# A fused kernel of linear attention and two MLPs: the decay chain laid out as fourteen steps of one slot, with ScalarE's cast of the hidden activations put ahead of it

## The chip, the cores and the metric

The kernel runs on one core of a Trainium2 chip, as one program with one instruction stream for each engine: PE (TensorE) multiplies matrices, DVE (VectorE), ACT (ScalarE) and POOL (GpSimd) work on rows of 128 partitions, and SP (SyncE) here only starts DMAs. The streams meet at semaphores. The metric is the device time of one execution in microseconds. Three runs of the kernel before gave 1022.08 us in the median (1019.12 to 1023.35).

## The reference

Three stages, all in fp32. The first is a recurrence over 768 tokens for 4 batches of 8 heads with a 48 x 48 state:

```python
mag = np.sqrt(a_re * a_re + a_im * a_im)
scale = np.minimum(mag, 0.999) / (mag + 1e-06)
a_re_n, a_im_n = (a_re * scale, a_im * scale)
for t in range(S):
    new_re = ar * S_re - ai * S_im
    new_im = ar * S_im + ai * S_re
    S_re, S_im = (new_re + kv, new_im)          # kv: outer product of k[t] and v[t]
    y[:, :, t] = np.einsum('bhd,bhde->bhe', q[:, :, t], S_re)
...
h = x @ w_in;  g = h * np.clip(h + 3.0, 0.0, 6.0) / 6.0;  x = g @ w_out      # 384 -> 2048 -> 384
a = x @ w1;  b = x @ w2;  out = ((a * b) @ w3) @ w_out2                       # 384 -> 1024 -> 1024 -> 384
```

## The kernel before, in words

**Units.** The 3072 tokens are 24 chunks of 128; three chunks are a unit of 384 tokens, so there are eight units (NU = 8) and six chunks to a batch. The recurrence is done by chunk: the decays of a token are turned into a magnitude and an angle, both are summed along the tokens, and q and k are multiplied by the exponential of the one sum and by the cosine and sine of the other. After that the scores of a chunk, its output y and the state's update are plain matrix products.

**Slots.** The first MLP sets the beat. A unit u >= 0 has sixteen slots, one for each 128 columns of the hidden layer (n = 16u + slot). In a slot PE does `gemm1(n)` (nine products into the bank `hb`), then `gemm2(n-2)` (nine products into `acc`). For each n ACT makes `t_sb` from `hb` (relu), DVE makes `g_sb`, ACT casts it to its high part `gH` (`high_g`), and POOL subtracts to get the low part `gL` (`low_g`). gemm2(n) needs both parts, gemm1(n+2) needs `g_sb` of n to have been made. `t_sb` and `g_sb` are single buffers; gH and gL have three.

**What rides on the slots.** Units -2 and -1 have no MLP work and fill the pipeline. The chunks of unit u+1 are treated in unit u, in three stages each: TK (PE transposes the rotated keys of a chunk; ACT and DVE copy them to `Kc` and `Ks`), S (`Sc`: scores from the tile `F`; DVE masks them) and YU (PE makes y and the state's update; ACT and DVE split y into high and low; SP stores it to `xHL`, six DMAs by L707 to L712). From unit 1 on they stand in slots 1, 5, 9 (TK), 2, 6, 10 (S) and 4, 8, 12 (YU). The last chunk of a batch has no TK and no update; it falls into the even units. The decay chain `pre(p, t)` of unit p, with t the step, is done in unit p-2: `steps(u, sl)` says which steps stand in which slot. It ends with `QKc` and `QKs`, q and k times the cosine and the sine. SP then scatters them by head into `F` with ten DMAs for the first two chunks (`scatter_pair`) and ten for the third (`scatter_last`, which writes where the first chunk stood).

**Order within a slot.** All engines walk the same two loops, and each does its slot's work in the order in which the code has it: an engine that waits holds up all that stands behind it, SP's DMAs too. On ACT, before: relu, the chain's step, `high_g`, the chunk's copies, the splits of weights. On DVE: `g_sb`, the chain's step, the chunk's work.

**Also in the pipeline's filling.** PE multiplies w3 by w_out2 in unit -2 (L890); ACT copies the eight blocks of rows out (`W3_COPY`) and SP stores them. The weights of the first MLP are split into high and low parts in eight pieces (`SPLIT_H` on ACT, `SPLIT_L` on POOL). In unit 7 the weights of the second MLP are split, each 3072 columns wide, on ACT (L1081) and DVE (L1279). After it comes the second MLP, which the change doesn't touch.

## Time and profile before

| | |
|---|---|
| median of three runs | 1022.08 us |
| the profiled execution, and its span | 1022.37 us, 1020.6 us |
| busy share of PE, DVE, ACT, POOL | 89%, 46%, 42%, 25% |
| mean granted TensorE clock | 0.946 of full speed |
| PE waited for F<-QKs, in total and times | 26.8 us, 8 |
| PE waited for POOL's gL in gemm2, in total and times | 23.6 us, 10 |

A busy share counts an instruction from its start to its end, and products overlap, so a high share of PE doesn't say that it runs at its best rate. What counts is the distance from one slot's first product to the next one's, against the same kind of slot where nothing was waited for. Everything else is read as lateness against that beat.

### The profile page before, as it was taken

How to read it: one execution, taken by the hardware profiler on the slowest of the kernel's cores; microseconds unless marked ns; L12 is line 12 of the kernel's file. 1: busy time of each engine (PE TensorE's matmuls, PEld its weight loads, DVE VectorE, ACT ScalarE, POOL GpSimd, SP SyncE). 2: the span in 40 equal slices, each digit the busy share in tenths (PEclk: the TensorE clock that was granted, in tenths of full speed). 3: DMA queues.
4: the chain of work that ended last, by engine and by line, in shares of the span. 5: the costliest groups of instructions: out<-in, count | busy, mean ns of one | idle time of the engine just before them, and what ended most of it. 6: DMA issues, size and time to landing. Idle time of an engine off the chain costs nothing.

```text
span 1020.6 us, 14665 instructions
## 1 busy us (share of the span) xinstructions
PE 910.4 (89%) x5721; PEld 834.9 (82%) x5721; DVE 470.5 (46%) x610; ACT 430.5 (42%) x650; POOL 256.6 (25%) x200
## 2 busy tenths in 40 slices
PE   6944469889989989989989989989999999999996
PEld 3534468879889889889889889989888888888886
DVE  6445549849658648648748733233212121212110
ACT  4543535555655655555555532353212122212121
POOL 1011336222222222222222222343222222222221
PEclk9977769989989999999999999999999999999999
DMA  9584132353343343343344141510101010101000
GB/s 347 201 230 128 46 63 78 85 119 88 108 87 95 100 91 98 93 90 99 107 89 110 48 84 50 188 68 11 44 1 62 1 62 1 62 1 62 1 32 33
DMA packets 73688, 85.85 MB, mean 84 GB/s; under 512 B 6928, under 2 KB 59792, under 8 KB 73616
## 3 DMA queue, kind: packets, MB, share of 16 engines
q1 hardware_dynamic: 73216, 84.07, 29.7%
q10 hardware_dynamic: 400, 0.80, 0.5%
q8 instruction: 48, 0.79, 0.3%
q14 instruction: 24, 0.20, 0.1%
HBM read 45.22 MB, written 11.01 MB: 55 GB/s over the span
## 4 chain that ended last, share of the span: by engine, by line
issue 39%; PE 38%; POOL 14%; DVE 3%; ACT 2%; DMA 2%; SPq 1%; ACTq 0%; POOLq 0%; DVEq 0%
POOL gL L1328 13%; PE hb L937 10%; PE acc L959 7%; PE bQ L937 5%; PE bR L937 5%; PE bP L959 2%; PE hb L796 2%; PE acc L816 2%; PE acc L890 2%; DMA F<-QKs 1%; PE hb L890 1%; DVE QKc L1198 1%; DMA wo_sb<-in_moe_w_out_dram 1%; PE bQ L846 0%; PE bR L846 0%
## 5 line engine op out<-in xcount | busy, mean ns | idle before, releaser
L1328 POOL TENSOR_TENSOR gL<-g_sb,gH 128x384 fp32r<-128x384 f32 x128 | 157.1, 1227 | 428.2 <-ACT gH L1036 425.9
L796 PE MATMUL hb<-xHL,winH 128*128 128x384 f32 x768 | 168.6, 356 | 10.7 <-DMA xHL<-yHL 9.1
L816 PE MATMUL acc<-gH,woutH 128*128 128x384 f32 x384 | 134.0, 349 | 32.5 <-POOL gL L1328 23.6
L1237 DVE SCALAR_TENSOR_TENSOR g_sb<-t_sb,hb 128x384 f32<-128x384 f32 x128 | 70.4, 550 | 189.6 <-ACT t_sb L1046 105.8
L796 PEld LDWEIGHTS hb<-xHL,winH 128*128 128x128 f32 x768 | 140.2, 199 | 13.3 <-DMA xHL<-yHL 9.5
L1046 ACT ACTIVATE t_sb<-hb,cst 128x384 f32<-128x384 f32 x128 | 74.4, 581 | 154.1 <-PE hb L796 153.4
L816 PE MATMUL acc<-gH,woutL 128*128 128x384 f32 x384 | 133.3, 347 | 0.0
L816 PE MATMUL acc<-gL,woutH 128*128 128x384 f32 x384 | 132.8, 346 | 0.0
L1341 POOL TENSOR_TENSOR pL<-p_sb,pH 128x512 fp32r<-128x512 f32 x48 | 67.0, 1396 | 231.9 <-ACT pH L1098 231.9
L816 PEld LDWEIGHTS acc<-gH,woutH 128*128 128x128 f32 x384 | 75.0, 195 | 37.6 <-issue 29.3
L1036 ACT CAST gH<-g_sb 128x384 fp32r<-128x384 f32 x128 | 65.3, 510 | 79.4 <-DVE g_sb L1237 79.2
L796 PE MATMUL hb<-xHL,winL 128*128 128x384 f32 x384 | 88.9, 339 | 0.0
L816 PEld LDWEIGHTS acc<-gH,woutL 128*128 128x128 f32 x384 | 75.4, 196 | 0.0
L816 PEld LDWEIGHTS acc<-gL,woutH 128*128 128x128 f32 x384 | 75.2, 196 | 0.0
L1090 ACT COPY a_sb<-hb 128x512 f32<-128x512 f32 x48 | 28.1, 586 | 102.7 <-PE hb L937 102.7
L796 PEld LDWEIGHTS hb<-xHL,winL 128*128 128x128 f32 x384 | 70.4, 192 | 0.0
L1296 DVE TENSOR_TENSOR p_sb<-a_sb,bQ 128x512 f32<-128x512 f32 x24 | 16.5, 688 | 110.2 <-PE bQ L937 94.4
L1098 ACT CAST pH<-p_sb 128x512 fp32r<-128x512 f32 x48 | 29.8, 621 | 85.5 <-DVE p_sb L1296 85.5
L1296 DVE TENSOR_TENSOR p_sb<-a_sb,bR 128x512 f32<-128x512 f32 x24 | 16.5, 686 | 104.7 <-PE bR L937 99.7
L846 PE MATMUL bQ<-F 128*128 128x128 f32 x192 | 32.5, 323 | 28.2 <-DMA F<-QKs 26.8
L846 PEld LDWEIGHTS bQ<-F 128*128 128x128 f32 x192 | 29.3, 228 | 31.9 <-DMA F<-QKs 29.7
L959 PE MATMUL acc<-woH,pL 128*128 128x384 f32 x144 | 48.7, 338 | 0.0
(148 smaller groups left out, 1715.9 us busy)
## 6 DMA issues: line engine op xcount, KB each, us to landing
QKs<-in_qk_x_dram SPq DMA_DIRECT2D x16, 576.0 KB, 4.2
xHL<-yHL SPq DMA_DIRECT2D x48, 144.0 KB, 2.7
F<-QKc SPq DMA_DIRECT2D x16, 292.5 KB, 4.7
AR<-in_a_re_x_dram SPq DMA_DIRECT2D x8, 576.0 KB, 3.9
...
```

Source lines behind the costliest of these rows:

```text
L796: mm = pe.matmul(o, w[:, kk * DF1 + ft * P:kk * DF1 + (ft + 1) * P], xv(u)[:, 2 * kk + part, :], start=(i == 0), stop=(i == 8))
L816: mm = pe.matmul(acc[m][:, 0:UNIT], w[:, ft * DM + m * P:ft * DM + (m + 1) * P], gg[:, (n % 3) * UNIT:(n % 3 + 1) * UNIT], start=(ft == 0 ...
L846: mm = pe.matmul(bk[:, hh * P:(hh + 1) * P], qk(f_of(g))[:, b, P:2 * P], qk(f_of(g))[:, b, 0:P], start=True, stop=True)
L890: mm = pe.matmul(w3_banks[i % nb][:, 0:DM], w3t_sb[:, j * DF2 + i * P:j * DF2 + (i + 1) * P], wo2_sb[:, j * DM:(j + 1) * DM], start=(j == ...
L937: mm = pe.matmul(bk[n % 2][:, :], w[:, kk * DF2 + ft * P:kk * DF2 + (ft + 1) * P], x[:, o:o + UNIT2], start=(i == 0), stop=(i == 8))
L959: mm = pe.matmul(acc2[tb][:, 0:DM], pp[:, o:o + P], w[:, ft * DM:(ft + 1) * DM], start=(ft == 0 and i == 0), stop=(ft == FT2 - 1 and i == 2))
L1036: act.copy(gH[:, (n % 3) * UNIT:(n % 3 + 1) * UNIT], g_sb[:, :]).then_inc(s["hswish_high"], 1)
L1046: act.activation(t_sb[:, :], hb[n % 2][:, 0:UNIT], ACT.Relu, bias=THREE_C).then_inc(s["relu_done"], 1)
L1237: dve.scalar_tensor_tensor(out=g_sb[:, :], in0=t_sb[:, :], scalar=6.0, in1=hb[n % 2][:, 0:UNIT], op0=ALU.min, op1=ALU.mult).then_inc(s["hs ...
L1296: dve.tensor_tensor(p_sb[:, (n % 2) * UNIT2:(n % 2 + 1) * UNIT2], a_sb[:, (n % 2) * UNIT2:(n % 2 + 1) * UNIT2], bb[n % 2][:, :], ALU.mult) ...
L1328: pool.tensor_tensor(gL[:, (n % 3) * UNIT:(n % 3 + 1) * UNIT], g_sb[:, :], gH[:, (n % 3) * UNIT:(n % 3 + 1) * UNIT].bitcast(F32), ALU.subt ...
L1341: pool.tensor_tensor(pL[:, (n % 3) * UNIT2:(n % 3 + 1) * UNIT2], p_sb[:, (n % 2) * UNIT2:(n % 2 + 1) * UNIT2], pH[:, (n % 3) * UNIT2:(n % ...
```

## The change

- **Steps.** The chain has fourteen steps (t = 0 to 13) in place of sixteen. From unit 1 on step t stands in slot t; slots 14 and 15 are empty. Work that an engine needs from the other one is made one slot earlier. The angle's arctangent is now at t = 6, ahead of the exponentials at t = 9, so that ACT changes its function table four times a chain, not three. The multiplication by 1/pi moves from ACT into three DVE instructions. A fourth work buffer `W4` is the room of `gH` for p < 2 and `x_sb` (x2_sb) after that, with waits that protect both.
- **Pair and last.** q and k of a unit are loaded, decayed and rotated in two portions: the first two chunks (`pair`), then the third (`last`). `scatter_pair` is issued for cosine and sine at t = 13, all of it from SP; before, at t = 14 and t = 15, and for p = 0 one half from ACT.
- **Loads.** The decay rows of the next unit (`load_a`) are asked for at t = 11, not t = 12 (slot 11 in place of slot 12 from unit 1 on).
- **ACT's order.** `high_g(n)` stands right behind the relu, ahead of the chain's step.
- **Splits.** The weight pieces are split in another order and other slots (`SPLIT_W`); w3's rows are copied out earlier; the splits in unit 7 are done in halves, one a slot.

```diff
-        SPLIT_H = {(-1, 0): (0,), (-1, 8): (4,), (-1, 9): (1,), (0, 1): (5,), (0, 3): (2,), (0, 5): (6,), (0, 7): (3,), (0, 9): (7,)}
+        SPLIT_W = {(-2, 15): (0,), (-1, 3): (1,), (-1, 8): (4,), (0, 0): (2,), (0, 2): (5,), (0, 4): (3,), (0, 6): (6,), (0, 8): (7,)}
...
             if u == -1:
-                return ([(1, 0)] if sl == 0 else []) + ([(1, sl + 1)] if sl < 9 else [])
+                return [(1, sl)] if sl <= 10 else []
             if u == 0:
-                return {0: [(1, 10), (1, 11)], 1: [(1, 12), (1, 13)], 2: [(1, 14), (1, 15)],
-                        3: [(2, 0), (2, 1)], 15: [(2, 13), (2, 14), (2, 15)]}.get(sl, [(2, sl - 2)])
-            return [(u + 2, sl)] if u + 2 < NU else []
+                return {15: [(2, 12), (2, 13)]}.get(sl, [(2, sl - 3)] if sl >= 3 else [(1, sl + 11)])
+            return [(u + 2, sl)] if u + 2 < NU and sl < 14 else []
...
-        W3_COPY = {(-2, 9): (0, 1), (-2, 10): (2,), (-2, 11): (3, 4), (-1, 0): (5,), (-1, 1): (6,), (-1, 2): (7,)}
+        W3_COPY = {(-2, 8): (0, 1), (-2, 9): (2,), (-2, 10): (3, 4), (-2, 14): (5, 6), (-2, 15): (7,)}
...
         def evac_x2_act(act, u):
...
+            act.wait_ge(s["turns_wrapped"], min(u + 3, NU))
...
         @block.sync
...
-                        if t == 12 and p + 1 < NU:
+                        if t == 11 and p + 1 < NU:
                             load_a(p + 1)
-                        if t == 14:
+                        if t == 13:
                             scatter_pair(sp, p, 0)
-                        if t == 15 and p > 0:
                             scatter_pair(sp, p, 1)
...
         @block.scalar
...
+                if t == 3:
+                    if p > 2:
+                        act.wait_ge(s["x2_stored"], 16 * KT * (p - 2))
+                    act.activation(W4(p)[:, :], W1[:, :], ACT.Exp, scale=-0.5).then_inc(s["exp_ln_mag"], 1)
...
+                if t == 6:
+                    act.wait_ge(s["atan_arg"], p + 1)
+                    act.activation(W2[:, :], W2[:, :], ACT.Arctan, scale=-1 / QUARTER_TURN).then_inc(s["atan_done"], 1)
+                if t == 9:
                     act.wait_ge(s["log_r_centred"], p + 1)
                     act.activation(mid_decay[:, :], blocks(W1)[:, :, P // 2 - 1], ACT.Exp).then_inc(s["mid_decays"], 1)
-                if t == 9:
-                    act.wait_ge(s["atan_num"], p + 1)
                     act.activation(AI[:, :], AR[:, :], ACT.Exp).then_inc(s["q_decays"], 1)
                     act.activation(AR[:, :], AR[:, :], ACT.Exp, scale=-1.0).then_inc(s["k_decays"], 1)
                 if t == 10:
-                if t == 12:
-                    act.wait_ge(s["turns_summed"], KT * (p + 1))
-                    act.mul(W2[:, :], W1[:, :], float(1 / np.pi)).then_inc(s["turns"], 1)
-                if t == 13:
                     act.wait_ge(s["turns_wrapped"], p + 1)
...
                         act.activation(t_sb[:, :], hb[n % 2][:, 0:UNIT], ACT.Relu,
                                        bias=THREE_C).then_inc(s["relu_done"], 1)
+                        high_g(n)
                         if sl == 1 and u > 0:
                             evac_x2_act(act, u - 1)
-                    if n is not None:
                         for p, t in steps(u, sl):
                             pre(p, t)
-                        high_g(n)
...
         @block.vector
...
                 if t == 12:
+                    dve.wait_ge(s["pair_decayed"], 2 * (p + 1))
                     dve.wait_ge(s["cos_turns"], p + 1)
                     for i in range(2):
-                        dve.tensor_tensor(part(QKc, i), part(QKs, i), tokens(W3), ALU.mult).then_inc(s["cos_rotated"], 1)
-                if t == 15:
+                        dve.tensor_tensor(pair(part(QKc, i)), pair(part(QKs, i)), pair(tokens(W2)), ALU.mult).then_inc(s["pair_cos"], 1)
...
-                    if u == NU - 1 and sl in (5, 7, 9):
+                    if u == NU - 1 and 4 <= sl < 10:
```

What this makes of the engines' order is shown at three places. First ACT in unit -2, the chain of unit 0 (W_64 and W_65 are work buffers, x_sb the place of w3's rows). Before:

```order
L1007 ACTIVATE W_64<-W_64 128x1152
L1010 ACTIVATE mid_decay<-W_63 128x9
L1013 ACTIVATE AI<-AR 128x1152
L1014 ACTIVATE AR<-AR 128x1152
L1075 COPY x_sb<-acc 128x384 x2
L1017 ACT_TABLE_LOAD
L1017 ACTIVATE W_64<-W_64 128x1152
L1075 COPY x_sb<-acc 128x384
```

and after it:

```order
L1022 ACTIVATE W_65<-W_65 128x1152
L1025 ACT_TABLE_LOAD
L1025 ACTIVATE W_65<-W_65 128x1152
L1086 COPY x_sb<-acc 128x384 x2
L1028 ACT_TABLE_LOAD
L1028 ACTIVATE mid_decay<-W_64 128x9
L1029 ACTIVATE AI<-AR 128x1152
L1030 ACTIVATE AR<-AR 128x1152
L1086 COPY x_sb<-acc 128x384
```

The arctangent (L1017, now L1025) has moved ahead of the first copies of w3's rows, and the two exponentials behind them, with a table load of their own. Second ACT in a steady unit. Before, slots 12 and 13 with the chain's end:

```order
L1020 ACTIVATE W_64<-W_63 128x1152
L1036 CAST gH<-g_sb 128x384
L1067 CAST yHL<-bP 128x4x128
L1046 ACTIVATE t_sb<-hb,cst 128x384
L1023 ACTIVATE W_64<-W_63 128x1152
L1025 ACT_TABLE_LOAD
L1025 ACTIVATE W_64<-W_63 128x1152
L1026 ACTIVATE W_64<-W_63 128x1152
```

After, slot 9 and the beginning of slot 10, the widest piece of the new chain:

```order
L1058 ACTIVATE t_sb<-hb,cst 128x384
L1048 CAST gH<-g_sb 128x384
L1028 ACT_TABLE_LOAD
L1028 ACTIVATE mid_decay<-W_64 128x9
L1029 ACTIVATE AI<-AR 128x1152
L1030 ACTIVATE AR<-AR 128x1152
L1070 COPY Kc<-bQ 128x288
L1071 COPY Kc<-bQ 128x2x32
L1072 COPY Kc<-bQ 128x2x16
L1058 ACTIVATE t_sb<-hb,cst 128x384
L1048 CAST gH<-g_sb 128x384
```

The cast to gH stood behind all of the chain's step and now stands ahead of it; the key copies Kc stand behind it in both. Third SP at the end of unit 1, the last chunk's stores (xHL), the decay rows (AR, AI) and the scatter. Before:

```order
L662 DMA v_sb_72<-in_v_dram 128x384
L707 DMA xHL<-yHL 48x6x128
L708 DMA xHL<-yHL 48x6x128
L709 DMA xHL<-yHL 32x2x128
L710 DMA xHL<-yHL 32x2x128
L711 DMA xHL<-yHL 16x2x128
L712 DMA xHL<-yHL 16x2x128
L640 DMA AR<-in_a_re_x_dram 128x1152
L640 DMA AI<-in_a_im_x_dram 128x1152
L338 DMA F_68<-QKc 48x2x780
```

and after it:

```order
L650 DMA AR<-in_a_re_x_dram 128x1152
L650 DMA AI<-in_a_im_x_dram 128x1152
L673 DMA v_sb_73<-in_v_dram 128x384
L720 DMA xHL<-yHL 48x6x128
L721 DMA xHL<-yHL 48x6x128
L722 DMA xHL<-yHL 32x2x128
L723 DMA xHL<-yHL 32x2x128
L724 DMA xHL<-yHL 16x2x128
L725 DMA xHL<-yHL 16x2x128
L347 DMA F_69<-QKc 48x2x780
```

The decay rows now go ahead of the last chunk's stores; the scatter stands directly behind these stores.

## Rows read from the trace of the kernel before

**Rows 1.** Windows, by unit: length, busy PE, PEld, DVE, ACT, POOL, clock, DMA share, GB/s

```profile
101.53:202.67 101.14, 74.21 (x490) 70.13 (x490) 67.80 (x76) 52.14 (x70) 40.84 (x22) 0.83 0.27 66
202.67:280.76 78.09, 70.64 (x531) 67.73 (x532) 51.07 (x68) 46.33 (x70) 18.66 (x16) 0.93 0.41 107
280.76:355.96 75.20, 69.39 (x509) 66.91 (x509) 51.79 (x68) 41.71 (x63) 20.19 (x17) 0.94 0.39 96
355.96:431.53 75.57, 70.08 (x531) 67.66 (x531) 51.37 (x69) 42.19 (x66) 19.29 (x16) 0.95 0.38 95
...
581.62:651.90 70.28, 67.07 (x509) 65.65 (x509) 24.19 (x41) 21.27 (x44) 16.57 (x16) 0.97 0.29 64
651.90:708.00 56.10, 51.95 (x287) 50.87 (x287) 18.98 (x20) 25.52 (x37) 23.63 (x16) 0.97 0.29 109
```

**Rows 2.** Timeline of PE, unit 2: first products of slots 4 to 7

```profile
302.47 1.20 PE L796 MATMUL hb<-xHL,winH 128*128 128x384 f32 x6
...
308.50 1.31 PE L796 MATMUL hb<-xHL,winH 128*128 128x384 f32 x6
...
312.30 1.29 PE L796 MATMUL hb<-xHL,winH 128*128 128x384 f32 x6
...
317.21 1.29 PE L796 MATMUL hb<-xHL,winH 128*128 128x384 f32 x6
```

**Rows 3.** Timeline of PE across the boundary of units 1 and 2

```profile
279.12 0.41 PE L816 MATMUL acc<-gH,woutH 128*128 128x384 f32 x1 [2.10 <-POOL gL L1328]
...
280.76 1.20 PE L796 MATMUL hb<-xHL,winH 128*128 128x384 f32 x6
...
283.88 1.20 PE L796 MATMUL hb<-xHL,winH 128*128 128x384 f32 x6
...
291.86 0.41 PE L816 MATMUL acc<-gH,woutH 128*128 128x384 f32 x1 [2.06 <-ACT gH L1036]
...
295.99 2.07 PE L846 MATMUL bQ<-F 128*128 128x128 f32 x8 [1.25 <-DMA F<-QKs]
```

**Rows 4.** Timeline of ACT, slot 13 of unit 1

```profile
272.47 1.28 ACT L1025 ACT_TABLE_LOAD   x1
273.77 1.26 ACT L1025 ACTIVATE W<-W,cst 128x1152 f32<-128x1152 f32 x1
...
277.39 0.51 ACT L1036 CAST gH<-g_sb 128x384 fp32r<-128x384 f32 x1
```

**Rows 5.** Timeline of DVE, slots 12 and 15 of unit 1

```profile
268.59 2.14 DVE L1188 TENSOR_TENSOR W<-W,W 128x1152 f32<-128x1152 f32 x1
...
283.38 3.43 DVE L1202 TENSOR_TENSOR QKs<-QKs,W 128x1152 f32<-128x1152 f32 x2
```

**Rows 6.** Timeline of SP, first and last of the ten scatters

```profile
283.02 0.60 SPq L338 DMA_DIRECT2D F<-QKc  x1
...
290.81 0.59 SPq L342 DMA_DIRECT2D F<-QKs  x1
```

**Rows 7.** Timelines of ACT, PE, SP and DVE, units -2 to 0

```profile
34.15 0.48 ACT L1075 COPY x_sb<-acc 128x384 f32<-128x384 f32 x1 [7.62 <-PE acc L890]
...
62.54 2.08 PE L846 MATMUL bQ<-F 128*128 128x128 f32 x8 [9.05 <-DMA F<-QKs]
63.83 7.41 SPq L697 DMA_DIRECT2D w3o_dram<-x_sb  x2
...
101.53 2.29 PE L796 MATMUL hb<-xHL,winH 128*128 128x384 f32 x6 [6.11 <-DMA xHL<-yHL]
...
124.16 5.84 DVE L1198 TENSOR_TENSOR QKc<-QKs,W 128x1152 f32<-128x1152 f32 x2
...
142.98 1.44 PE L846 MATMUL bQ<-F 128*128 128x128 f32 x5 [3.94 <-DMA F<-QKs]
```

**Rows 8.** Timelines of POOL and PE in unit 7

```profile
681.29 3.50 POOL L1328 TENSOR_TENSOR gL<-g_sb,gH 128x384 fp32r<-128x384 f32 x1 [3.28 <-ACT gH L1036]
...
684.93 0.66 PE L816 MATMUL acc<-gH,woutH 128*128 128x384 f32 x1 [2.38 <-POOL gL L1328]
```

More of the change, by code:

```diff
@@ L259, in rows_of, with half @@
             return t[:, :].rearrange("p (c j n) -> p j c n", j=KT, n=QK)
+        def half(t, i):
+            n = N1 // 2
+            return t[:, i * n:(i + 1) * n]
         def hd(t):
@@ L719, in _ @@
                 if j == 3:
[L720 to L721 removed]
+                    load_pair(0)
+                    load_last(0)
             for i in range(2):
@@ L753, in _ @@
                         load_x2(0)
-                    if u == NU - 2 and sl == 15:
+                    if u == NU - 2 and sl == 13:
                         for i in range(2):
@@ L1075, in _ @@
                         act.copy(x2_sb[:, (i % 3) * DM:(i % 3 + 1) * DM], w3_banks[i % len(w3_banks)][:, 0:DM]).then_inc(s["w3_row_copied"], 1)
-                    for i in SPLIT_H.get((u, sl), ()):
+                    for i in SPLIT_W.get((u, sl), ()):
                         split_H(act, i)
-                    if u == NU - 1 and sl in (4, 6, 8):
-                        i = sl // 2 - 2
+                    if u == NU - 1 and 3 <= sl < 9:
+                        i, part2 = divmod(sl - 3, 2)
                         act.wait_ge(s[f"mlp2_w_dma{i}"], 16)
-                        act.copy(w2parts[i][0][:, :], w2parts[i][2][:, :]).then_inc(s["mlp2_w_high"], 1)
+                        act.copy(half(w2parts[i][0], part2), half(w2parts[i][2], part2)).then_inc(s["mlp2_w_high"], 1)
             split_x2_act(act, 0)
@@ L1166, in pre @@
                     dve.tensor_copy(fs, fc).then_inc(s["f_column"], 1)
-                if t == 10:
-                    dve.wait_ge(s["q_decays"], p + 1)
-                    dve.wait_ge(s["q_dma"], 16 * (p + 1))
-                    dve.tensor_tensor(part(QKs, 0), part(QKs, 0), tokens(AI), ALU.mult).then_inc(s["q_decayed"], 1)
+                    dve.wait_ge(s["k_decays"], p + 1)
+                    dve.wait_ge(s["pair_dma"], 16 * (p + 1))
+                    for i, grow in enumerate((AI, AR)):
+                        dve.tensor_tensor(pair(part(QKs, i)), pair(part(QKs, i)), pair(tokens(grow)), ALU.mult).then_inc(s["pair_decayed"], 1)
@@ L1193, in pre @@
-                if t == 14:
-                    dve.wait_ge(s["q_decayed"], p + 1)
-                    dve.wait_ge(s["k_decayed"], p + 1)
+                    dve.wait_ge(s["last_dma"], 16 * (p + 1))
+                    for i, grow in enumerate((AI, AR)):
+                        dve.tensor_tensor(last(part(QKs, i)), last(part(QKs, i)), last(tokens(grow)), ALU.mult).then_inc(s["last_decayed"], 1)
+                if t == 12:
+                    dve.wait_ge(s["pair_decayed"], 2 * (p + 1))
                     dve.wait_ge(s["cos_turns"], p + 1)
@@ new lines, in pre, with pair @@
+                if t == 13:
+                    dve.wait_ge(s["last_decayed"], 2 * (p + 1))
+                    for i in range(2):
+                        dve.tensor_tensor(last(part(QKc, i)), last(part(QKs, i)), last(tokens(W2)), ALU.mult).then_inc(s["last_cos"], 1)
+                    for i in range(2):
+                        dve.tensor_tensor(last(part(QKs, i)), last(part(QKs, i)), last(tokens(W3)), ALU.mult).then_inc(s["last_sin"], 1)
+            def pair(v_):
+                return v_[:, :, 0:2, :]
@@ L1204, in part, with last @@
+            def last(v_):
+                return v_[:, :, 2, :]
             def part(t_, i):
@@ L1336, in _ @@
                         low_g(n)
-                    for i in SPLIT_L.get((u, sl), ()):
+                    for i in SPLIT_W.get((u, sl), ()):
                         split_L(pool, i)
```

172 lines of the change are left out of this document (87 added, 85 removed).

## The prediction, made before the changed kernel ran

> **What bounds the kernel now.** I read the windows by unit first [rows 1]. Each row is one unit of sixteen slots: its length, the busy time of each engine, the granted clock as a share of full speed. The rows are those of units 0 to 3, 6 and 7; units 4 and 5 read like 2 and 3. Unit 0 takes 101 us, units 1 to 5 some 75 to 78, unit 6 70, unit 7 56. PE is busy for nine tenths of a steady unit, yet DVE for 51 us and ACT for 42 of some 75: neither is full, so what is lost is lost to lateness, not to capacity.
>
> How much is lost I read off PE's beat [rows 2]. A slot with YU lasts 308.50 - 302.47 = 6.03 us, one with TK 3.80, one with S 4.91; a plain one 283.88 - 280.76 = 3.12 [rows 3]. Seven plain slots and three of each other kind give 21.8 + 44.2 = 66.1 us. In the even units one chunk has no TK (0.7 us) and no state update, which I estimate at 0.9 of YU's 2.9 us: 64.5. Against [rows 1] the loss is 12.0 us in unit 1, 10.7 in unit 2, 9.5 in unit 3, some 10 and 9.5 in units 4 and 5, 5.8 in unit 6: 57.5 us. Unit 7 has no riders, so 49.9 us would do, against 56.1: 6 us.
>
> Where it is lost stands in [rows 3]: gemm2 waits 2.10 us for gL at the end of unit 1 and 2.06 us for gH in slot 1 of unit 2, and S in slot 2 waits another 1.25 us for F. The clock is 0.93 to 0.95 in these units against 0.97 in units 6 and 7 [rows 1]: after these waits PE works a while at the lower level, and that goes with the loss.
>
> The first wait is ACT's order: a table load at 272.47, cosine, sine, a second load, and only at 277.39 the cast to gH [rows 4]. The last one is SP's: the rotation by the sine begins at 283.38 [rows 5], the ten scatters go from 283.02 to 291.40 (8.4 us), and F is there 4.6 us after that, at 295.99 [rows 6, 3].
>
> In the pipeline's filling [rows 7], ACT sits idle 7.6 us until w3's first row is summed, with unit 0's arctangent behind it; F comes at 62.54; SP then stands 7.4 us at w3's last stores with scatter_last and the x store queued behind; gemm1 starts at 101.53; the first score of unit 0 has its F at 142.98.
>
> **The change, part by part, in units 1 to 6.** *Cast first.* The two waits for gL and gH go, each with its stretch of lower clock. What is late next is the chain itself: ACT now waits in each slot for g before it may start its step, some 0.6 us (relu's end to DVE's end).
>
> *Scatter.* Before, the scatter began 2.3 us into slot 0 of the next unit, 9.4 + 2.3 = 11.7 us after slot 13 began. Now pair's rotations stand in slot 12. From slot 13's start: DVE done with them at +2.7, with y's low half at +3.3, six x stores as on any chunk (0.65 us apart) until +7.2, ten scatters +15.6, landed +20.2. S in slot 2 wants F at 5 x 3.12 + 3.80 = +19.4. So F is 0.8 us late rather than hidden by a wide margin, and it moves with DVE's lateness. I take 1.5 us with clock, from 0 to 4.
>
> *Chain work in ten dense slots.* DVE's chain is about as long as before and now lies in slots 3 to 10 and 12. A two-input product of 1152 columns takes 1.35 us alone and 2.14 beside POOL's gL [rows 5]. Taking 0.75 for a one-input instruction and 2.7 for three scans, as estimates from that 1.35, the chain's work in slots 4 to 8 is 3.5 + 2.7 + 3.4 + 2.7 + 2.9 = 15.2 us, the chunks' some 5 and g 2.4, with up to 4 for POOL: 23 to 27 us, where PE's beat takes 6.03 + 3.80 + 4.91 + 3.12 + 6.03 = 23.9. So DVE may be 0 to 3 us late in slot 9.
>
> *Slot 9 of the odd units.* From slot 9's start: nine products 1.6, relu 0.6, g 0.55, cast 0.5, that is +3.3; then table load 1.28 [rows 4], a short exponential 0.2, two long ones 2.3, key copies 0.7: +7.8. S in slot 10 wants the copies at 3.80 + 3.12 = +6.9. That is at least 0.9 us late; with DVE's lateness up to 4. I take 3.5 us with the lower clock that follows. The even units have no TK there and are spared. This fourth table load is new: it takes 1.28 us, and the next instruction starts 1.30 us after it began [rows 4]. The Trainium skill (ScalarE: Activation LUTs, What ACT_TABLE_LOAD costs) puts a switch at 1.28 us plus 1.38 us of draining, 2.66 us; the row shows nothing of the second part. By the page the copies would come 1.4 us later, 4 us more over three odd units.
>
> So a steady odd unit should last 66.1 + 5 = 71 us, an even one 64.5 + 2.5 = 67, unit 6 67. Unit 1 is worse: its chain's last steps (2, 12) and (2, 13) still share slot 15 of unit 0, DVE needs 5.3 us for them, F lands some 14 us into unit 1 and is wanted at 10: 66.1 + 6 + 3.5 = 75.6. Gains: 2.5 + 8.2 + 4.5 + 7.5 + 4.5 + 3.3 = **30.5 us**.
>
> **Unit 7.** While DVE splits 3072 columns POOL's gL takes 3.50 us, and PE waits 2.38 us for it [rows 8]; two more such places cost less. A half takes half as long and one gL fits behind it in each slot: g 0.5, half split 1.7, gL 1.0 is 3.3 us a slot against 3.12, six times, inside the buffers' slack. I take **5 us** of the 6. By the Trainium skill (SBUF — State Buffer, Who interferes with whom) whichever of the two starts first holds the shared ports for the whole instruction; the row fits, and it is also why more DVE instructions in the dense slots can hold up gL.
>
> **Filling.** Unit 0's chain: the arctangent is out of the way before ACT's 7.6 us of idleness; from 34.15 follow two row copies, load, exponentials (38.9), abs, load, cosine (43.2), copies, sine (45.3). SP can start scattering at 45.0, but all ten go from one queue: 53.2, landed 57.8 against 62.54. 4.7 us earlier. PE's w3 products end at 52 and don't stand in the way. Unit -1: w3's stores no longer stand ahead of scatter_last, so x of chunk 0 is stored 8 us earlier; DVE's steps stand between key copies and masks and give back 1.5: gemm1 starts at about 95, **6.6 us** earlier. Unit 0: before, the cosine product took 5.84 us for two, behind POOL's weight piece [rows 7], and F came 41.5 us after gemm1 began. Now the arctangent, exponentials and cosine of unit 1 precede relu(0); sine, load and one weight piece follow; DVE's pair rotations start at 107, wait for POOL's piece split at 106 (3.4 us), end at 114; scatters until 119.6, landed 124.3 in place of 142.98: 18.7 us earlier in all, **12.1 us** beyond gemm1's 6.6. The rest of unit 0 gains perhaps **2 us**.
>
> **Sum.** 30.5 + 5 + 6.6 + 12.1 + 2 = 56.2 us. The span 1020.6 becomes 964.4; the profiled execution's own time was 1.8 us above its span: 966. That execution took 1022.37 us, the median is 1022.08, so 966 stands as it is.
>
> **Costs at nothing.** ACT's wait in slot 3 for x2_stored: x2 is copied out in slot 1 and stored in slot 2, on HBM some 5 us later, about when slot 3's step begins. SP has ended its scatters at +15.6, and slot 1 begins at +12.5, so the store could be 3 us late; then ACT is, with relu(4) behind it, and still inside the slack of some 3 us between gL and gemm2. The load of the decay rows is needed five slots on.
>
> **Rivals.** *(B) The lateness only moves.* DVE runs over in slots 4 to 9, key copies and F both come 3 to 4 us late with stretches of lower clock, and units 1 to 6 gain under 12 us. For it: DVE's 51 us in a 66 us unit, in bursts; a margin for F of less than nothing. Against: before, slots 3 to 12 kept the beat with nearly the same load. Then 1022 - 12 - 5 - 15 = 990, from 980 to 1002. *(C) All of it goes.* Units 1 to 6 within 1.5 us of the beat, unit 1 within 5: gain 57.5 - 12.5 = 45, and 5 + 25 besides: 947, from 938 to 952. For it: before, the late engine always caught up in the plain slots. *(D) Slower.* With the cast first, the loop relu, g, gH, ACT's step, next relu contains DVE's step as well whenever DVE is late, since ACT may not start its step before g. Were both steps fully in series, a unit would take 1.64 x 16 = 26 us for the loop, some 27 of ACT's and some 45 of DVE's work: 98 us in place of 75, 23 more in each of five units, 1022 - 32 + 115 = 1105. It decides from the point where units 1 to 6 lose over 32 us together, 5 a unit, that is where a third of the two engines' work no longer overlaps. Against: PE's gemm1 gives relu its input two slots ahead of need. *(E) No change worth the name*: filling and steady units cancel.
>
> **Chances.** Forecast (952 to 979) 0.60, B 0.18, C 0.15, D 0.04, E 0.03. The forecast's unknowns are the key copies (0.9 to 4 us, three times), F (0 to 4 us, six times), DVE in unit 0 (6 us either way). For 8 in 10 I take most of C's upper half and B's lower half: 946 to 988. Faster by over 0.5%, which is about what a measurement of this kernel can tell from no change, 0.94; within 0.5% 0.02; slower 0.04.
>
> **What would show it.** Right: slots 15 and 1 of the units without a wait for gL or gH; the scatters beginning about 7 us into slot 13; F no more than 2 us late in slot 2; a wait for Kc in slot 10 in units 1, 3 and 5 and none in 2 and 4; F at about 58 and 124 us; gemm1 at 95; unit 7 under 52 us; no POOL gL over 2 us there. Wrong: waits for gL in slots 9 to 12 (B), ACT waiting for x2_stored in slot 3, units of over 76 us (D), or units 2 and 4 at 65 (C).

## The result, and the profile after

Four runs of the changed kernel gave 983.14 us in the median (982.52 to 984.38), beside 1022.27 us for the kernel before: a ratio of 0.9624, 95% interval 0.9600 to 0.9647. It is 39 us faster; 56 were forecast. The profiled execution took 984.38 us with a span of 982.5.

The windows by unit, cut at gemm1's first products as [rows 1] are; the last row runs to the first product of the second MLP:

```profile
100.08:192.04 91.96, 72.17 (x491) 68.41 (x491) 69.00 (x84) 53.78 (x71) 39.34 (x21) 0.87 0.29 72
192.04:267.16 75.12, 68.67 (x530) 66.05 (x531) 58.07 (x82) 41.62 (x65) 19.95 (x16) 0.98 0.44 112
267.16:338.18 71.02, 67.14 (x509) 63.46 (x509) 53.60 (x73) 41.56 (x63) 20.46 (x17) 1.00 0.40 101
338.18:410.24 72.06, 67.01 (x530) 64.38 (x530) 53.18 (x75) 42.22 (x66) 20.08 (x17) 1.00 0.40 101
...
554.45:620.86 66.41, 65.19 (x508) 63.77 (x509) 20.18 (x38) 21.31 (x44) 16.12 (x17) 1.00 0.32 69
620.86:674.05 53.19, 53.19 (x307) 52.89 (x307) 21.26 (x25) 28.07 (x43) 22.66 (x17) 1.00 0.30 113
```

Against the starts of the units before, the gains are 1.45 us up to gemm1's start (6.6 forecast), 9.2 in unit 0 (14.1 forecast), 3.0, 4.2, 3.5, 3.2, 2.7 and 3.9 in units 1 to 6 (2.5, 8.2, 4.5, 7.5, 4.5, 3.3), and 6.6 in unit 7 (5), where the same stretch took 711.71 - 651.90 = 59.81 us before.

PE's waits, whole program (what PE waited for, from whom: us in total, times, longest):

```profile
PE bQ L859 <- DMA F<-QKs: 23.6, 8, 8.1
...
PE hb L809 <- DMA xHL<-yHL: 11.6, 5, 5.6
...
PE hb L809 <- DVE g_sb L1261: 7.8, 4, 2.6
PE bQ L859 <- ACT Kc L1072: 7.7, 5, 1.8
...
PE acc L829 <- POOL gL L1352: 1.4, 1, 1.4
```

The waits for gL, 23.6 us before, are gone but for one, and others have grown: for g itself (1.6 us before), for Kc (1.0), for the x store (9.1). At the end of unit 2 they look like this (timeline of PE, slots 13 to 15 of unit 2, slot 0 and S in slot 2 of unit 3; the counterpart of [rows 3]):

```profile
324.74 1.33 PE L809 MATMUL hb<-xHL,winH 128*128 128x384 f32 x6
...
328.18 1.31 PE L809 MATMUL hb<-xHL,winH 128*128 128x384 f32 x6
...
333.53 1.33 PE L809 MATMUL hb<-xHL,winH 128*128 128x384 f32 x6 [1.72 <-DVE g_sb L1261]
...
338.18 1.33 PE L809 MATMUL hb<-xHL,winH 128*128 128x384 f32 x6 [0.91 <-DMA xHL<-yHL]
...
349.83 1.16 PE L859 MATMUL bQ<-F 128*128 128x128 f32 x8 [1.30 <-DMA F<-QKs]
```

Slots 14 and 15 last 5.35 and 4.65 us where 3.12 would do. Behind it stand these rows of ACT, slots 9 to 12 of unit 2 (for [rows 4]):

```profile
309.92 0.59 ACT L1058 ACTIVATE t_sb<-hb,cst 128x384 f32<-128x384 f32 x1 [1.03 <-PE hb L809]
313.57 0.51 ACT L1048 CAST gH<-g_sb 128x384 fp32r<-128x384 f32 x1 [3.06 <-DVE g_sb L1261]
314.10 1.28 ACT L1028 ACT_TABLE_LOAD   x1
315.40 0.22 ACT L1028 ACTIVATE mid_decay<-W 128x9 f32<-128x9 f32 x1
...
317.63 0.56 ACT L1058 ACTIVATE t_sb<-hb,cst 128x384 f32<-128x384 f32 x1
...
326.95 0.58 ACT L1058 ACTIVATE t_sb<-hb,cst 128x384 f32<-128x384 f32 x1
```

and these of DVE, the rotations of the pair in slot 12, y's low half and g(13) (for [rows 5]), and of SP, the first and the last scatter (for [rows 6]):

```profile
312.99 0.55 DVE L1261 SCALAR_TENSOR_TENSOR g_sb<-t_sb,hb 128x384 f32<-128x384 f32 x1
...
328.04 2.64 DVE L1209 TENSOR_TENSOR QKc<-QKs,W 128x768 f32<-128x768 f32 x2
330.61 1.81 DVE L1212 TENSOR_TENSOR QKs<-QKs,W 128x768 f32<-128x768 f32 x2
332.34 0.68 DVE L1290 TENSOR_TENSOR yHL<-bP,yHL 128x512 fp32r<-128x512 f32 x1
332.94 0.53 DVE L1261 SCALAR_TENSOR_TENSOR g_sb<-t_sb,hb 128x384 f32<-128x384 f32 x1
```

```profile
337.01 0.60 SPq L347 DMA_DIRECT2D F<-QKc  x1
...
344.45 0.60 SPq L351 DMA_DIRECT2D F<-QKs  x1
```

ACT had made relu(9) by 310.5, but its wait for g stands ahead of its own step: DVE is at that time in the step of slot 8 and makes g(9) at 312.99, so the exponentials start at 315.4 and relu(10) comes at 317.63. In slot 12 the rotations then lie between g(12) and y's low half.

Of the filling and unit 0 (timelines of PE, SP and DVE, the counterparts of [rows 7]):

```profile
35.85 9.44 SPq L710 DMA_DIRECT2D w3o_dram<-x_sb  x5
...
62.15 2.08 PE L859 MATMUL bQ<-F 128*128 128x128 f32 x8 [8.12 <-DMA F<-QKs]
...
112.94 5.03 DVE L1209 TENSOR_TENSOR QKc<-QKs,W 128x768 f32<-128x768 f32 x2
...
130.83 2.08 PE L859 MATMUL bQ<-F 128*128 128x128 f32 x8 [6.50 <-DMA F<-QKs]
```

In unit 7 no gL takes longer than the 1.92 us of this row of POOL (3.50 in [rows 8]):

```profile
649.71 1.92 POOL L1352 TENSOR_TENSOR gL<-g_sb,gH 128x384 fp32r<-128x384 f32 x1 [1.28 <-ACT gH L1048]
```

### The profile page after: what moved, and what is told of

The parts are those of the page before. It is cut to its first block, busy times and chain, and to the rows that moved or that the text cites. A ratio compares the mean times of both kernels' runs of the same rounds, so it can differ in the third digit from the quotient of the medians.

```text
span 982.5 us, 14750 instructions
## 1 busy us (share of the span) xinstructions
PE 892.5 (91%) x5721; PEld 815.1 (83%) x5721; DVE 490.4 (50%) x669; ACT 431.4 (44%) x653; POOL 263.2 (27%) x200
## 4 chain that ended last, share of the span: by engine, by line
PE 46%; issue 25%; POOL 10%; DVE 7%; ACT 4%; SPq 4%; DMA 3%; POOLq 0%; DVEq 0%; ACTq 0%
PE hb L950 10%; POOL gL L1352 9%; PE acc L972 8%; PE acc L829 5%; PE hb L809 5%; PE bQ L950 5%; PE bR L950 5%; PE bP L972 3%; DMA F<-QKs 2%; PE acc L903 2%; PE hb L903 1%; SPq L349 1%; DVE g_sb L1261 1%; DVE QKc L1209 1%; PE bQ L859 1%
## 5 line engine op out<-in xcount | busy, mean ns | idle before, releaser
L1352 POOL TENSOR_TENSOR gL<-g_sb,gH 128x384 fp32r<-128x384 f32 x128 | 160.3, 1253 | 387.5 <-ACT gH L1048 383.6
L809 PE MATMUL hb<-xHL,winH 128*128 128x384 f32 x768 | 164.8, 350 | 19.5 <-DMA xHL<-yHL 11.6
L809 PEld LDWEIGHTS hb<-xHL,winH 128*128 128x128 f32 x768 | 134.1, 192 | 24.7 <-DMA xHL<-yHL 13.3
L829 PE MATMUL acc<-gH,woutH 128*128 128x384 f32 x384 | 130.4, 339 | 2.5 <-POOL gL L1352 1.4
L829 PE MATMUL acc<-gH,woutL 128*128 128x384 f32 x384 | 129.4, 337 | 0.0
L829 PE MATMUL acc<-gL,woutH 128*128 128x384 f32 x384 | 129.3, 337 | 0.0
L829 PEld LDWEIGHTS acc<-gL,woutH 128*128 128x128 f32 x384 | 73.0, 190 | 0.0
L829 PEld LDWEIGHTS acc<-gH,woutL 128*128 128x128 f32 x384 | 72.8, 190 | 0.0
L859 PE MATMUL bQ<-F 128*128 128x128 f32 x192 | 29.3, 300 | 31.4 <-DMA F<-QKs 23.6
L859 PEld LDWEIGHTS bQ<-F 128*128 128x128 f32 x192 | 26.3, 208 | 35.6 <-DMA F<-QKs 26.0
```

Of the source, the lines that this page charges most:

```text
L809: mm = pe.matmul(o, w[:, kk * DF1 + ft * P:kk * DF1 + (ft + 1) * P], xv(u)[:, 2 * kk + part, :], start=(i == 0), stop=(i == 8))
L829: mm = pe.matmul(acc[m][:, 0:UNIT], w[:, ft * DM + m * P:ft * DM + (m + 1) * P], gg[:, (n % 3) * UNIT:(n % 3 + 1) * UNIT], start=(ft == 0 ...
L859: mm = pe.matmul(bk[:, hh * P:(hh + 1) * P], qk(f_of(g))[:, b, P:2 * P], qk(f_of(g))[:, b, 0:P], start=True, stop=True)
L1352: pool.tensor_tensor(gL[:, (n % 3) * UNIT:(n % 3 + 1) * UNIT], g_sb[:, :], gH[:, (n % 3) * UNIT:(n % 3 + 1) * UNIT].bitcast(F32), ALU.subt ...
```

## The experiments

The ratios are to the kernel before, run on the same chip. Names of tiles and engines are those of the kernel as told above.

**The cast, put back.** In the changed kernel only ACT's order is undone:

```diff
-                        high_g(n)
                         if sl == 1 and u > 0:
                             evac_x2_act(act, u - 1)
                         for p, t in steps(u, sl):
                             pre(p, t)
+                        high_g(n)
```

> The changed kernel, with the cast to gH put back behind the chain's step. Theory: with the dense steps the cast is late in slots 9 (load and two exponentials, 3.8 us) and 10 (3.7 us), and the slack between gL and gemm2 is some 3 us; 1 to 2 us with the lower clock at each, 2 to 4 us a unit in units 0 to 5: 995 us, from 990 to 1005, and PE waits for gL over 12 us in all (1.4 now). Rival: the steps are short enough for the cast to stand where it did: 983 us within 2, and the gain of the steady units came from the scatter alone.

Measured: 959.57 us, ratio 0.9405 (0.9381 to 0.9429). Both forecasts fall: with the cast in its old place the kernel is faster, so its new place costs more than it brings, 0.9624 - 0.9405 = 0.0219 of 1022 us, 22 us. Units 2, 3 and 4 last 65.18, 69.30 and 65.68 us in place of 71.02, 72.06 and 71.16, unit 0 86.16 in place of 91.96, and PE waits for gL once, 2.2 us, and for gH once, 2.3 us: the waits that the early cast was to remove are gone without it too. (Another 2.0 us of the trace's difference arose before gemm1, where the edit does nothing.) Timeline of ACT in this kernel, the same slots 9 to 12 of unit 2:

```profile
299.70 0.58 ACT L1058 ACTIVATE t_sb<-hb,cst 128x384 f32<-128x384 f32 x1 [1.49 <-PE hb L809]
300.31 1.28 ACT L1028 ACT_TABLE_LOAD   x1
...
304.24 0.57 ACT L1058 ACTIVATE t_sb<-hb,cst 128x384 f32<-128x384 f32 x1
...
312.11 0.57 ACT L1058 ACTIVATE t_sb<-hb,cst 128x384 f32<-128x384 f32 x1
```

From relu(9) to relu(12) it takes 312.11 - 299.70 = 12.4 us, against 326.95 - 309.92 = 17.0 with the cast first. The step of slot 9 runs here while DVE is still in that of slot 8. What ACT waits for g over unit 2, in the changed kernel and in this one (us in total, times, longest):

```profile
ACT gH L1048 <- DVE g_sb L1261: 25.2, 16, 3.9
...
ACT gH L1048 <- DVE g_sb L1261: 12.8, 7, 2.8
```

**Only the wait.** This parts two readings of the 22 us: that ACT's step waits for g, or that the earlier gL of POOL falls beside DVE's products. The cast is behind the step again, its wait for g is left ahead of it:

```diff
-                        high_g(n)
+                        act.wait_ge(s["hswish"], n + 1)
                         if sl == 1 and u > 0:
                             evac_x2_act(act, u - 1)
                         for p, t in steps(u, sl):
                             pre(p, t)
+                        high_g(n)
```

> The changed kernel with the cast behind the chain's step, as in the run of 959.6 us, but with ACT's wait for g left ahead of the step. Theory (the loop): what costs 24 us is not where the cast stands but that ACT may not begin its step before DVE has made g, and DVE makes g only behind its own step of the slot before, so the two engines' steps no longer overlap. Then this kernel is as slow as the changed one, or slower, since gL comes later too: 983 us or more. Rival (the ports): the early cast sends POOL's gL beside DVE's products, and it is that contention which costs; the cast is late here, so 960 to 965 us. In between, 970 to 978: both.

Measured: 985.84 us, 0.9658 (0.9626 to 0.9690), as slow as the changed kernel, and units 2 to 4 of 71.86, 72.03 and 71.71 us. Timeline of ACT, slot 9 of unit 2:

```profile
312.64 1.28 ACT L1028 ACT_TABLE_LOAD   x1
315.69 0.22 ACT L1028 ACTIVATE mid_decay<-W 128x9 f32<-128x9 f32 x1 [1.76 <-DVE g_sb L1262]
```

With the cast late the wait alone costs 985.84 - 959.57 = 26 us; with the wait there, the early cast of the changed kernel makes 3 us at most (0.9624 beside 0.9658, intervals that overlap). So the wait makes the price, and an early gL beside DVE's products isn't needed for it. Only ACT's table load (312.64) starts here before g is made; the first exponential stands until 315.69. The slots that are late are not all the same ones: PE waits for gL 7.2 us in all here (1.4 in the changed kernel), and slot 12 of units 2 and 4 lasts 7.7 us for 5.4, slot 14 3.8 for 5.4.

**The cast first, alone, in the kernel before.**

```diff
+                        high_g(n)
...
                     if n is not None:
                         for p, t in steps(u, sl):
                             pre(p, t)
-                        high_g(n)
```

> The kernel before, with nothing changed but the cast to gH ahead of the chain's step. Theory (a wait takes the place of the one removed): PE's waits for gL and gH at the units' boundaries, 23.6 us for gL in all, go, but the scatter is where it was, so PE comes to slot 2 earlier and waits there for F some 4 to 5 us in place of 1.25; little is won: 1015 to 1021 us. Rival (the two are worth their own price each): the boundaries win 3 to 4 us each, five times: 1005 us, with F's waits under 2 us. Second rival: the chain's step waits for g in each slot and DVE for it in turn: slower than 1024 us.

Measured: 1042.36 us, 1.0223 (1.0199 to 1.0247): slower by 23 us. That is the time that the second rival gave. PE's waits in this kernel:

```profile
PE hb L796 <- DVE g_sb L1237: 19.5, 6, 4.3
PE acc L816 <- ACT x_sb L409: 14.7, 6, 3.4
PE bQ L832 <- DVE QKc L1198: 13.3, 1, 13.3
...
PE acc L816 <- POOL gL L1328: 5.8, 8, 2.4
```

gL's waits fall from 23.6 to 5.8 us as forecast, and three others grow by more: before, they were 1.6 us for g, none for x_sb and 3.9 for QKc. ACT waits for g 128 times here, 205.2 us in all (82 times and 79.2 us before). So the order costs about as much, 22 to 23 us, with the old steps as with the new ones; that it is the wait here too was not tried by itself.

**Rotations over three slots** (the changed kernel, cast first):

```diff
-            return [(u + 2, sl)] if u + 2 < NU and sl < 14 else []
+            return [(u + 2, sl)] if u + 2 < NU and sl < 15 else []
...
+                if t == 13:
                     dve.wait_ge(s["sin_turns"], p + 1)
                     for i in range(2):
                         dve.tensor_tensor(pair(part(QKs, i)), ...
-                if t == 13:
+                if t == 14:
                     dve.wait_ge(s["last_decayed"], 2 * (p + 1))
```

> The changed kernel, with the rotations over three slots on DVE: pair by the cosine in slot 12 as now, pair by the sine in slot 13, the third chunk in slot 14 (it shared slot 13). Theory: in slot 12 four rotations of 4.4 us stand between g and y's low half, so y low is 1.8 us late, six x stores and ten scatters behind it on SP too, and g(13) comes late. Then in units 2 and 4 slots 14 and 15 (5.35 and 4.65 us) come back to 3.12 each, 3.7 us a unit, and slot 2 of units 1 to 6 (6.4 to 6.6 us) to about 5.0, 1.5 us each: 983 - 7.4 - 9 = 967 us, from 966 to 975. Rival (SP's sixteen DMAs of 0.65 us set F's time, not DVE): slot 2 stays at 6.4 to 6.6 us, and at most the slots 14 and 15 win: 976 us or more. Second rival: the third chunk one slot later is late for the next chain (AR and AI, scatter_last): 983 or more.

Measured: 976.53 us, 0.9576 (0.9554 to 0.9598). That is 5 to 6.6 us less than the changed kernel where 16 were expected, and in the range of the first rival. Slot 2 of unit 2 comes to 4.93 us and slot 14 to 3.6, but slot 15 stays at 4.6, with a wait of 0.99 us for the x store behind it, and in the odd units slot 2 keeps 6.6 to 8.2 us. So the rotations' place accounts for a part only.

**The cast put back and the rotations spread**, both edits as above:

> The changed kernel with the cast behind the chain's step and the rotations in three slots (two edits that gave 959.6 us and 976.5 us by themselves). Theory: they don't add up, since part of what the rotations gave was in slots 14 and 15 of the even units, where the first edit leaves 3.1 and 3.4 us already; what is left is F in slot 2 (11.97, 5.01, 6.71, 5.51, 7.67 and 5.63 us in units 1 to 6, against 4.91): 1.8 us in unit 3, 3 to 4 in unit 5, 0.6 in units 4 and 6, nothing in unit 1, whose chain ends in slot 15 of unit 0: 953 us, from 951 to 957. Rival: SP's sixteen DMAs set F's time, so nothing is left to gain: 959 within 1.5.

Measured: 953.75 us, 0.9340 (0.9312 to 0.9368), as expected. Windows of this kernel, units 2 and 3:

```profile
261.22:326.02 64.80, 64.80 (x510) 63.70 (x510) 51.07 (x73) 41.24 (x63) 18.58 (x16) 1.00 0.42 106
326.02:393.70 67.68, 66.33 (x531) 64.44 (x531) 51.89 (x76) 42.19 (x67) 18.79 (x16) 1.00 0.46 112
```

Unit 2 has PE busy throughout; 64.80 us is what I had estimated as the beat of an even unit (64.5). Units 4 and 6 last 64.80 too.

**The roundings behind the state update**, on top of the kernel before this one:

```diff
+                if (t, p > 2) in ((8, False), (8.5, True)):
                     dve.wait_ge(s["turns_summed"], KT * (p + 1))
                     dve.tensor_scalar(W2[:, :], W4(p)[:, :], float(1 / np.pi), ROUND, ...
...
+                    if 0 < u < NU - 2 and sl == 8:
+                        pre(u + 2, 8.5)
```

> As the kernel before it in this call, and with the two roundings of step t = 8 on DVE behind the chunk's y low and state update in slot 8 of units 1 to 5. Theory: TK in slot 9 of units 1, 3 and 5 waits some 1.4 us for bR, which DVE's state update reads behind 3.7 us of the chain's step; with 2.3 us fewer ahead of it slot 9 comes from 5.27 to 3.9 us there: 4 us less than the kernel without it, 949 us. Rival: DVE is only busy in another order, and g(9), which comes 2.3 us behind the state update now, makes the exponentials and the key copies later: no gain, or a loss of 1 to 3 us.

Measured: 952.22 us, 0.9317 (0.9285 to 0.9348): by the times not to be told from 953.75. By the trace slot 9 of the odd units comes from 5.25 to 3.80 us, slot 10 from 4.93 to 5.10, and unit 3 from 67.68 to 66.34 (66.1 estimated). These two are the fastest kernels here, 29 and 31 us below the changed one.

**Fewer exponentials ahead of Kc.** The third one goes behind the key copies:

```diff
-                    act.activation(AR[:, :], AR[:, :], ACT.Exp, scale=-1.0).then_inc(s["k_decays"], 1)
+                    if p < 3:
+                        act.activation(AR[:, :], AR[:, :], ACT.Exp, scale=-1.0).then_inc(s["k_decays"], 1)
...
+                    if u > 0 and (u + 2, 9) in steps(u, sl):
+                        act.activation(AR[:, :], AR[:, :], ACT.Exp, scale=-1.0).then_inc(s["k_decays"], 1)
```

> The changed kernel, with the last of the three exponentials of step t = 9 behind the key copies Kc on ACT, from unit 1 on. Theory: in units 1, 3 and 5 S waits 1.8 us in slot 10 for Kc, because table load and exponentials (3.8 us) stand ahead of the copies; slot 10 lasts 6.95 us where S costs 4.91. With 1.15 us fewer ahead of the copies the wait falls to 0.7 us and below and slot 10 to 5.3 or so: 1.5 us in each of three units, 978.5 us, from 977 to 981. Units 2, 4 and 6, without key copies there, are as before. Rival: DVE's Ks copies end as late as ACT's (they stand behind its step t = 9), so the wait only changes its name: 983 within 1.

Measured: 984.68 us, 0.9653 (0.9611 to 0.9696), no gain. Slot 10 of units 1, 3 and 5 did come from 6.95 to 5.90 us (5.3 expected), but their slot 15 went from 3.12, 3.26 and 3.48 to 4.00, 4.32 and 4.02: what one slot wins is given back five slots on. I put that down to the loop of relu, g and step, which is still late; no run shows that step by itself. With the cast put back the same slot 10 lasts 4.91 us with nothing else changed.

**The sine's scatter from ACT.**

```diff
                             scatter_pair(sp, p, 0)
-                            scatter_pair(sp, p, 1)
...
+                if t == 13:
+                    scatter_pair(act, p, 1)
```

> The changed kernel, with the five scatters of the sine's half issued by ACT (at t = 13, of every unit) and only the cosine's five by SP. Theory Q (SP's queue sets F's time): the last scatter is issued 3.3 us earlier in each unit, F lands 3 us earlier, slot 2 of units 1 to 6 comes from 6.5 to 4.9 us, 1.6 us each, and unit 0's F and unit -1's first score come some 3 us earlier: 983 - 9.6 - 5 = 968 us, from 966 to 976. Theory L (what comes late is DVE's and ACT's own work): ACT's five issues of 0.6 us hold up its relu and cast in slots 13 and 14, PE waits there what it saves in slot 2: 980 to 988 us.

Measured: 1015.85 us, 0.9962 (0.9936 to 0.9987), 33 us slower than the changed kernel. Slot 2 of units 2 to 6 did come to 4.93 us, so the queue's half of the theory holds, but slot 15 went to 7.8 to 11.5 us. Timelines of SP, ACT and PE at the end of unit 2:

```profile
339.51 2.18 SPq L722 DMA_DIRECT2D xHL<-yHL  x1
341.73 1.95 SPq L723 DMA_DIRECT2D xHL<-yHL  x1
...
340.06 1.78 ACTq L349 DMA_DIRECT2D F<-QKs  x1
341.87 1.84 ACTq L350 DMA_DIRECT2D F<-QKs  x1
...
344.70 0.58 ACT L1059 ACTIVATE t_sb<-hb,cst 128x384 f32<-128x384 f32 x1 [5.51 <-issue]
...
350.20 2.29 PE L808 MATMUL hb<-xHL,winH 128*128 128x384 f32 x6 [7.80 <-DMA xHL<-yHL]
```

The scatter now runs beside the x stores, which gemm1 needs first; their issues take 2.18 and 1.95 us in place of 0.6, and ACT's relu stands 5.5 us. Which of the two costs more I did not part.

**Without most of POOL's splits in unit 0.** This kernel leaves out nearly all of the low parts of five weight pieces; PE takes the high part of these weight pieces in the place of the low one.

```diff
-            eng.tensor_tensor(piece(i, winL, woutL), piece(i, winL_raw, woutL_raw), ...
+            c = slice(0, None if i in (0, 1, 4) else 8)
+            eng.tensor_tensor(piece(i, winL, woutL)[:, :, c], piece(i, winL_raw, woutL_raw)[:, :, c], ...
...
+                        w = winH if ft >= 8 else w
...
+                        w = woutH if ft >= 4 else w
```

> The changed kernel without most of POOL's low parts of the weight pieces 2, 3, 5, 6 and 7 (8 columns of each are made), PE taking the high part in the place of the low one, so the result lacks these products' low share; PE's work is the same. Theory: POOL's splits in unit 0 (some 4.3 us each) stretch what DVE does beside them (a one-input instruction of 0.75 us takes 4.0 us at relu(0), another 3.4 us in slot 8), and the stretch stands on unit 0's path three to four times: unit 0 from 92.0 to 84 us or less, F of unit 1 by 3 us or more earlier; 983 - 8 = 975 us, from 970 to 978. Rival: unit 0 is bound by the chain of unit 1's own length and SP's order; then F comes 1 us earlier at most and the whole wins under 3 us: 980 us or more.

Measured: 978.98 us, 0.9587 (0.9545 to 0.9629), some 4 us less than the changed kernel, with intervals that overlap; plainer is unit 0 in the trace, 86.57 us in place of 91.96, with slot 8 of 6.34 us in place of 9.70. The two cosine rotations of unit 1, which took 5.03 us beside POOL's split of 3.46 us, take here:

```profile
113.00 2.64 DVE L1212 TENSOR_TENSOR QKc<-QKs,W 128x768 f32<-128x768 f32 x2
```

So POOL's splits make 5.4 us of unit 0's length, between theory and rival. The Trainium skill (SBUF — State Buffer, Who interferes with whom) calls the port pair that DVE and GpSimd share an exclusive lock; the pair of rows agrees: the split held POOL from 112.03 to 115.49 us, DVE's first product was begun at 112.94, and the two took 2.4 us more.

**The filling.** Steps t = 5 to 10 of unit 1's chain behind the last chunk's work:

```diff
-                return [(1, sl)] if sl <= 10 else []
+                return {5: [], 6: [], 7: [], 8: [], 9: [(1, 5), (1, 6)], 10: [(1, 7), (1, 8)], 11: [(1, 9), (1, 10)]}.get(
+                    sl, [(1, sl)] if sl < 5 else [])
```

> The changed kernel, with steps t = 5 to 10 of unit 1's chain put behind the last chunk's work in unit -1 (two a slot in slots 9, 10 and 11). Theory: of the filling's gain of 6.6 us that I had forecast only 1.5 came, because DVE's steps t = 5 and t = 6 stand ahead of the last chunk's key copies and masks; PE waits 2.7 us for the masks there. Without them the first score is masked 4 us earlier and gemm1 starts 2.5 to 4 us earlier, at 96 to 97.6 us; the chain of unit 1 itself is 3 to 5 us later, relu(0) and F behind it too, so unit 0 gives most of that back: 980 to 985 us in all. Rival: the last chunk is held by what stands ahead of it (scatter_last, the x stores); then gemm1 starts at 99 to 101 us, as now.

Measured: 990.56 us, 0.9706 (0.9677 to 0.9735). PE of this kernel, its first two slots that wait:

```profile
96.41 2.29 PE L810 MATMUL hb<-xHL,winH 128*128 128x384 f32 x6 [5.62 <-DMA xHL<-yHL]
...
112.52 2.29 PE L810 MATMUL hb<-xHL,winH 128*128 128x384 f32 x6 [10.24 <-DVE g_sb L1262]
```

gemm1 starts 3.7 us earlier, as the theory has it; but then PE stands 10.24 us, since relu(0) comes behind the chain's moved steps, and unit 0 lasts 100.72 us. I had underrated what it gives back.

**Two more.** The halves of unit 7 alone, in the kernel before (both splits by `half(...)` over slots 3 to 9, as in the change):

> The kernel before, with nothing changed but unit 7's splits of the second MLP's weights, in halves, one a slot. Theory: all that unit 7 gained in the changed kernel (59.8 to 53.2 us from its first product to that of the second MLP) comes from the halves. Then this kernel takes 1022.3 - 6.6 = 1015.7 us, units 0 to 6 are as before within 0.5 us each, and unit 7's slots last 3.12 us. Rival: part of it came from what stands ahead (unit 6 hands over in a better state, the loads of the weights are asked for two slots earlier). Then it takes 1018 us or more and some slot of unit 7 lasts over 3.5 us.

Measured: 1011.32 us, 0.9934 (0.9910 to 0.9959), that is 6.7 us (4.2 to 9.2) less. Unit 7 takes 53.18 us, its slots 0 to 14 3.12 each: for unit 7 that is the theory. Its other half, units 0 to 6 as before within 0.5 us, did not hold in the trace: units 2 to 5 were 1.1 to 2.3 us shorter each than in the trace of before, which no edit explains; runs of the kernel before spread over 1017.0 to 1024.8 us beside it.

The output weights' loads moved on SP from slot 0 to slot 2 of unit -1:

```diff
-                    if u == -1 and sl == 0:
+                    if u == -1 and sl == 2:
```

> The changed kernel, with the loads of the output weights' four pieces two slots later in unit -1 (3 MB, asked for right behind the last stores of w3's rows and unit 0's scatter). Theory: they take the DMA engines from the scatter's small packets, so that F lands 6.65 us after its last issue where it takes 4.6 in the steady units; without them F of unit 0 comes at 60 us in place of 62.15, and gemm1 starts 1 to 2 us earlier: 981.5 us, from 980.5 to 982.5. Rival: F's time is its own, the two us aren't there: 983 within 0.7. Second rival: the pieces come too late for their split in slots 8 of unit -1 and 2 of unit 0: over 984 us.

Measured: 984.11 us, 0.9648 (0.9604 to 0.9691). It tested nothing: SP has no other work in those slots, so the loads were asked for at 55.51 us, straight behind w3's stores, as before. Whether they delay F stays open.

## Why the prediction was right, and where it was wrong

The time lies in the range of 946 to 988 us and the sign is right, but it is outside the forecast's own 952 to 979 and in the band of rival B, and it is there for neither's reason. Units 1 to 6 gained 20.5 us where 30.5 were forecast and B had under 12; the filling and unit 0 gained 10.7 for 20.7, unit 7 6.6 for 5. That the range held is in part luck: it was widened for a lateness of DVE, and what filled it is the mechanism of D, which was given 0.04 and only as a kernel slower than before.

*Cast first* is the step that failed. I had it as a gain ("the two waits for gL and gH go"), with "some 0.6 us" of waiting a slot as its only price. The waits did go, but they go without it too (2.2 us for gL and 2.3 for gH with the cast put back): the rest of the change removed them. What the early cast itself made is a price of 22 us. It is the mechanism of rival D: ACT's step may not begin before g, g stands on DVE behind DVE's last step, so the two engines' steps follow each other in place of overlapping. My words against it, that relu has its input two slots ahead, were beside the point: not relu but the step has to wait. Told by unit: over unit 2, ACT waited for g 16 times and 25.2 us, which is 1.6 us a slot and not 0.6; with the cast put back it was 7 times and 12.8 us. I had also set the point of decision where D becomes slower than before, and did not ask what the loop costs below it. That point is also off: D takes 32 us for what the other parts gain, and their terms make 5 + 6.6 + 12.1 + 2 = 25.7, so it lies at a loss of 26 us in units 1 to 6, 4.3 a unit. Without the early cast the change gains not 39 but 39 + 22 = 61 us, where 56 were forecast with it. Of these 61, unit 7's halves were tried alone (6.7 us); how the rest divides between the new steps, the pair and the order of the loads was not parted.

*Units 1 to 6.* Forecast 75.6, 67, 71, 67, 71, 67; measured 75.1, 71.0, 72.1, 71.2, 73.1, 66.4. Units 1 and 6 are right by the number; in unit 1 F came 14.8 us after its start (14 forecast), but PE was late itself and waited 1.75 us for it, not 4. The odd ones are near it by terms that are not those I named alone: slot 10 waits 1.8 us for Kc, as said, but another 1.45 us are lost in slot 9, where TK waits for the state update behind DVE's roundings (the kernel with these behind it has 3.80 us there). In the even units, for which the forecast adds 2.5 us and names a term for only 1.5 of them, I had taken DVE and ACT for spared, having no TK in slot 9. They are not: PE runs ahead there, and relu(12), the rotations and g(13) come late in slots 14 and 15, 3.8 us. F was late by 1.1 to 1.4 us (1.75 in unit 1, 2.1 in unit 5), about as given, and the scatter, forecast about 7 us into slot 13, began 265.83 - 257.69 = 8.1 us into slot 13 of unit 1, but 337.01 - 324.74 = 12.3 into that of unit 2, behind y's low half.

*Beat and clock.* The beats were right: with the order put right, units last 64.80 and 66.34 us (64.5 and 66.1 estimated). I had added lower clock to each wait; but the clock of units 2 to 7 of the changed kernel is 1.00, waits of 0.9 to 2.1 us and all.

*Filling.* F of pair 0 came at 62.15, not 57.8: w3's first row was there at 35.35, not at 34.15, SP stood at w3's five stores until 45.3, and F landed 6.65 us after SP had issued the last scatter (55.50) where I had taken 4.6. So the first chunk was hardly earlier, and its x store, forecast 8 us earlier, came 3.3 us earlier (75.26 for 78.57): I had counted all of SP's 7.4 us of waiting [rows 7] as gain, but scatter_last needs the first chunk's y as well and went at 67.47 for 71.29. The other 1.85 us of the 3.3 I put down to steps t = 5 and 6, close to the 1.5 given. With steps 5 to 10 behind, gemm1 starts 3.7 us earlier, 1 us of which is F's (61.10).

*Unit 0.* F came 30.75 us after gemm1's start where I had 29.3, and 2.3 us of that is POOL's split under the rotations (128.50 without it): a gain of 10.7 us for 12.1. The rest of the unit, forecast 2 us shorter, was 1.5 us longer: slot 8 lasts 9.70 us (5.89 before, 6.34 without the splits), with PE waiting 2.83 us for Ks behind steps of DVE that a split stretches.

*Unit 7* gained 6.6 us for 5, its mechanism confirmed alone.

*Costs at nothing.* ACT waits nowhere for x2_stored, and no wait for AR or AI is new. Of the signs that were to show the forecast wrong, none appeared: no wait for gL in slots 9 to 12 from unit 1 on, no unit of 76 us from there on, and none of 65. Of those that were to show it right, the waits of slots 15 and 1, of slot 10 and unit 7's gL came as said; F (62.15 and 130.83 for 58 and 124) and gemm1 (100.08 for 95) did not. None watched for what happened, a loop that is late without stopping PE at gL.

*Table loads.* The load that the change adds costs what the rows say: in unit 2 it starts at 314.10 us, takes 1.28, and the next instruction starts 1.30 after it began. The Trainium skill (ScalarE: Activation LUTs, What ACT_TABLE_LOAD costs) adds 1.38 us of draining; no run here shows it.
